# Attention inside a fused attention and MLP kernel: from split single-pass matmuls with transposes and repeated denominators to plain f32 matmuls on array tiles

## The chip, the cores and the metric

One core of a Trainium2 chip runs the whole program. The metric is the time of one execution on the device in microseconds (us), as the median of several executions. Less is better.

## What is computed

For 8 batches and 8 heads of 576 tokens with 64 values each, the reference computes an attention with 128 exponential features and their inverses, and then two MLP blocks:

```python
def phi(x):
    proj = np.einsum('bhsd,df->bhsf', x, w_phi)
    proj = proj - np.max(np.abs(proj), axis=-1, keepdims=True)
    return np.concatenate([np.exp(proj), np.exp(-proj)], axis=-1)
q_p, k_p = (phi(q), phi(k))
kv = np.einsum('bhsf,bhsd->bhfd', k_p, v)
z = np.sum(k_p, axis=2)
num = np.einsum('bhsf,bhfd->bhsd', q_p, kv)
den = np.einsum('bhsf,bhf->bhs', q_p, z)[..., None] + 1e-06
x = num / den                       # heads side by side: 8 x 576 x 512
# block 1: token shift with mu_k, mu_r; k = relu(xk @ w_k); v = (k * k) @ w_v; x = sigmoid(xr @ w_r) * v
# block 2: h = relu(x @ w_in); 3-tap convolution, sigmoid gate; out = (h * gate) @ w_out
```

All arrays are float32.

## The kernel before

**Two phases.** Phase 1 computes the attention and the first MLP block of all eight batches, and stores its result y to the chip's memory. Phase 2 (`phase_2`) reads it back and computes the second block. The change touches phase 1 alone.

**Numbers as pairs.** Nearly every large product is made of three matmuls (`three`): an operand is split into a high part of type f32r, which TensorE streams in one pass, and the low rest. Only the product of the keys' features with v (`sum_kv`, step KV) runs as plain f32.

**The attention of a pair of heads.** A batch has four pairs p. The steps of one pair are, by their letters in the lists of steps: T turns q and k (`turn`, ten TensorE transposes into the PSUM tensor `ps0`, then ACT writes the high and DVE the low part); QP and KP project q and k on all features with tokens on the partitions (`project`), and DVE takes the maxima of the magnitudes (`max_q`, `shift_k`; the second also subtracts them); M turns the split maxima of q into rows of `ps1` (`turn_maxima`), and ACT copies them; PA and PB make the features of q of one head each, with the features on the partitions, in `ps1` (`feature_rows`), and ACT takes both exponentials; SA and SB split them; EK takes the exponentials of k; KV sums the keys' features times v and 1; NA and NB multiply with the features of q (`attend`), again in `ps1`, where one row is the denominator. ACT copies numerator and denominator row out (`copy_num`).

**The denominators.** A row of 2 x 576 denominators goes by a transfer to a 128 x 9 tile, is inverted there (step RC, `invert`), goes to memory, and is read back repeated on 64 partitions for each head. Step DV (`divide`) multiplies on DVE and writes `x`.

**The first MLP block.** For each half of the tokens (288 of 576) there are 8 tiles K, 4 tiles R and 4 tiles V; a K or R tile is 12 matmuls, a V tile is two steps of 12 (`V-` and `V`). Their PSUM banks are the three of `psm`, in turn. Steps XK, HK, LK and XR, HR, LR mix and split x for them (group 0 is the first three pairs, group 1 the last pair).

**The order of the work.** Each engine runs one list of steps in order and waits on semaphores. `first_attention_steps` is the list for the first batch's attention, which has no MLP work beside it. `iteration` writes the list for one batch's MLP mixed with the next batch's attention: after an attention step it adds tiles worth so many ns (`FILL_NS`, `FIRST_FILL`, `TURN_FILL`) by the estimates of `PE_NS`; steps RC and DV follow NB by `RC_AFTER` and `DV_AFTER` ns of the same count, and are put in behind the step that passes that time. `batches` runs the first attention, one mixed iteration, a loop of six more, and the last MLP.

Of the kernel before, what the change touches and what calls it, by code (L numbers as in the profile page):

```python
# [11 lines left out]
P = 128  # L22
# [12 lines left out]
VW = D + 2  # L35
# [21 lines left out]
def attention_steps():  # L57

    steps = [("T", 0), ("QP", 0)]
    for p in range(PAIRS):  # L60
        more = p + 1 < PAIRS
        steps += [(s, p) for s in ("KP", "M", "EK", "PA", "SA", "KV", "PB")]
        steps += [("T", p + 1)] if more else []
        steps += [("SB", p), ("NA", p)]
        steps += [("QP", p + 1)] if more else []
        steps += [("NB", p)]
    return steps


def first_attention_steps():  # L70

    steps = [("T", 0), ("QP", 0), ("KP", 0)]
    for p in range(PAIRS):
        last = p == PAIRS - 1

        def ahead(s):
            return [(s, 0, "next") if last else (s, p + 1)]

        def before(s):
            return [(s, p - 1)] if p else []  # L80

        steps += [("M", p)] + before("RC") + [("PA", p), ("SA", p), ("EK", p)] + ahead("T")
        steps += [("PB", p)] + before("DV") + [("SB", p), ("KV", p)] + ahead("QP") + [("NA", p)]
        if not last:
            steps += ahead("KP") + [("NB", p)]
        else:
            steps += [("XK", 2, 0), ("NB", p), ("HK", 2, 0), ("LK", 2, 0), ("RC", p)]
            steps += [("XR", 2, 0), ("HR", 2, 0), ("LR", 2, 0)] + ahead("KP") + [("DV", p)]
    return steps + [(s + w, 2, 1) for w in "KR" for s in "XHL"]
# [6 lines left out]
def iteration(with_moe, with_next, ran_ahead=False):  # L96
# [38 lines left out]
    if with_next:  # L135
        fill(FIRST_FILL)
        for step in attention_steps():
            s, p = step[:2]
            if not (ran_ahead and step in (("T", 0), ("QP", 0), ("KP", 0))):
                emit(step)  # L140
            if with_moe:
                fill(FILL_NS.get(s, 0))
                if s == "NB":
                    later += [(now + RC_AFTER, ("RC", p)), (now + DV_AFTER, ("DV", p))]
                    later.sort(key=lambda t: t[0])
                if (s, p) in (("T", 0), ("PB", PAIRS - 1), ("NA", PAIRS - 1)):
                    fill(TURN_FILL * (2 if s == "NA" else 1))
        if with_moe:
            end = max(at for at, step in later if step[0] == "DV")
# [27 lines left out]
def build(nc, q, k, v, w_phi, mu_k, mu_r, w_k, w_v, w_r, w_in, conv_w, w_out, out):  # L177
    den_scr = nc.dram_tensor("den_scr", (PAIRS, 2, S), F32, kind="Internal").ap()
# [3 lines left out]
    with ExitStack() as ctx:  # L182
        early = phase_1(nc, ctx, q, k, v, w_phi, mu_k, mu_r, w_k, w_v, w_r, y_scr, den_scr, w_in)
# [26 lines left out]
def phase_1(nc, ctx, q, k, v, w_phi, mu_k, mu_r, w_k, w_v, w_r, y_scr, den_scr, w_in):  # L210
# [16 lines left out]
    phi_hi, phi_lo = sb_att("phi_hi", [P, 2, F], F32R), sb_att("phi_lo", [P, 2, F], F32R)  # L227
    ident = sb_att("ident", [P, P])
    pick = sb_att("pick", [P, 2, F], F32R)

    qk_nat = sb_att("qk_nat", [P, 2, TT, 2 * D])
    v_nat = sb_att("v_nat", [P, TT, 2, VW])
    qk_hi, qk_lo = sb_att("qk_hi", [P, 2, TT * P], F32R), sb_att("qk_lo", [P, 2, TT * P], F32R)
    q_max, k_max = sb_att("q_max", [P, TT, 2]), sb_att("k_max", [P, TT, 2])
    q_max_split = sb_att("q_max_split", [P, TT, 2, 2], F32R)
    max_rows = sb_att("max_rows", [P, TT * P], F32R)
    k_shift = sb_att("k_shift", [P, TT, 2, F])
    k_exp = sb_att("k_exp", [P, TT, 2, F])

    pick_f = k_exp[:, 0, :, :]  # L240
    phi = k_exp[:, 1, :, :]
    q_exp = sb_att("q_exp", [P, 2, S])
    q_exp_hi, q_exp_lo = sb_att("q_exp_hi", [P, 2, S], F32R), sb_att("q_exp_lo", [P, 2, S], F32R)
    kvz = sb_att("kvz", [P, 2, 2, 2 * D])
    kvz_hi, kvz_lo = sb_att("kvz_hi", [P, 2, 2, 2 * D], F32R), sb_att("kvz_lo", [P, 2, 2, 2 * D], F32R)
    num = sb_att("num", [P, S])
    den_row = sb_att("den_row", [1, 2, S])
    den_cols = sb_att("den_cols", [P, 2 * S // P])
# [32 lines left out]
    kv_summed, kvz_copied, kvz_hi_ready, kvz_lo_ready = sem("kv_summed"), sem("kvz_copied"), sem("kvz_hi_ready"), sem("kvz_lo_ready")  # L281
    features = sem("features")
# [946 lines left out]
```

## Time and profile before

| | us |
|---|---|
| median of the runs shown | 1486.46 (1486.41 to 1493.02) |
| span of the profiled execution, first to last instruction | 1483.8 |
| TensorE busy | 1416.3 (95%) |
| DVE busy | 818.5 (55%) |
| ACT busy | 797.9 (54%) |
| POOL busy | 14.4 (1%) |

The profiled execution has no time of its own beside its span; the median of the runs lies 2.7 us above that span. Matmuls are pipelined, so the busy time of one in a row counts its whole way through the array; how many fit in a microsecond is read from the distance between starts.

### The profile page before, as it was taken

How to read it: one execution, taken by the hardware profiler on the slowest of the kernel's cores; microseconds unless marked ns; L12 is line 12 of the kernel's file. 1: busy time of each engine (PE TensorE's matmuls, PEld its weight loads, DVE VectorE, ACT ScalarE, POOL GpSimd, SP SyncE). 2: the span in 40 equal slices, each digit the busy share in tenths (PEclk: the TensorE clock that was granted, in tenths of full speed). 3: DMA queues.
4: the chain of work that ended last, by engine and by line, in shares of the span. 5: the costliest groups of instructions: out<-in, count | busy, mean ns of one | idle time of the engine just before them, and what ended most of it. 6: DMA issues, size and time to landing. Idle time of an engine off the chain costs nothing. (4 is left out here: it accounts for less than half of the span.)

```text
span 1483.8 us, 26980 instructions
## 1 busy us (share of the span) xinstructions
PE 1416.3 (95%) x10240; PEld 1362.4 (92%) x10240; DVE 818.5 (55%) x1141; ACT 797.9 (54%) x1400; POOL 14.4 (1%) x20
## 2 busy tenths in 40 slices
PE   5778999999999999999999999999889999999998
PEld 5778999999999999999999999999879889988997
DVE  4565555554645564465555555554386468456653
ACT  4656674674666557466565746755244344344442
POOL 0000000000000000000000000000110000000000
PEclk9999999999999999999999999999999999999999
DMA  4412202211120221212122022121201110110101
GB/s 125 126 31 57 58 17 65 69 30 50 45 61 26 57 61 30 66 41 49 38 61 58 17 66 66 27 91 46 72 34 61 68 40 22 67 60 16 51 28 36
DMA packets 153461, 77.42 MB, mean 52 GB/s; under 512 B 131728, under 2 KB 140048, under 8 KB 152336
## 3 DMA queue, kind: packets, MB, share of 16 engines
q1 hardware_dynamic: 153360, 75.91, 18.5%
q8 instruction: 83, 1.36, 0.4%
q14 instruction: 18, 0.15, 0.0%
HBM read 56.71 MB, written 19.02 MB: 51 GB/s over the span
## 5 line engine op out<-in xcount | busy, mean ns | idle before, releaser
L512 PE MATMUL psm<-xk_hi,wk_hi 128*128 128x288 f32 x512 | 153.4, 300 | 16.5 <-DVE xk_lo L885 12.0
L1047 PE MATMUL psh<-y_hi,win_hi 128*128 128x288 f32 x512 | 154.0, 301 | 13.5 <-ACT h L1132 9.1
L1048 PE MATMUL psh<-y_lo,win_hi 128*128 128x288 f32 x512 | 152.5, 298 | 0.0
L512 PE MATMUL psm<-k_hi,wv_hi 128*128 128x288 f32 x512 | 152.1, 297 | 0.0
L1049 PE MATMUL psh<-y_hi,win_lo 128*128 128x288 f32 x512 | 151.9, 297 | 0.0
L512 PE MATMUL psm<-xk_lo,wk_hi 128*128 128x288 f32 x512 | 151.7, 296 | 0.0
L512 PE MATMUL psm<-xk_hi,wk_lo 128*128 128x288 f32 x512 | 151.2, 295 | 0.0
L512 PE MATMUL psm<-k_lo,wv_hi 128*128 128x288 f32 x512 | 151.1, 295 | 0.0
L512 PE MATMUL psm<-k_hi,wv_lo 128*128 128x288 f32 x512 | 150.8, 295 | 0.0
L890 DVE TENSOR_TENSOR k_lo<-square,k_hi 128x288 fp32r<-128x288 f32 x128 | 58.6, 458 | 156.1 <-ACT square L740 155.6
L1190 DVE SCALAR_TENSOR_TENSOR conv<-h,taps,conv 128x576 f32<-128x576 f32 x64 | 55.2, 863 | 141.7 <-ACT conv L1134 141.7
L844 DVE TENSOR_TENSOR q_exp_lo<-q_exp,q_exp_hi 128x1152 fp32r<-128x1152 f32 x60 | 81.5, 1359 | 88.4 <-ACT q_exp_hi L709 88.4
L512 PEld LDWEIGHTS psm<-xk_hi,wk_hi 128*128 128x128 f32 x512 | 96.8, 189 | 18.4 <-issue 10.1
L1047 PEld LDWEIGHTS psh<-y_hi,win_hi 128*128 128x128 f32 x512 | 97.2, 190 | 16.3 <-ACT h L1132 11.4
L1132 ACT ACTIVATE h<-psh 128x576 f32<-128x576 f32 x64 | 41.8, 653 | 129.6 <-DVE gated L1178 94.3
L1049 PE MATMUL pso<-wout_hi,g_lo 128*128 128x512 f32 x256 | 101.1, 395 | 0.0
L1047 PE MATMUL pso<-wout_hi,g_hi 128*128 128x512 f32 x256 | 101.0, 395 | 0.0
L1048 PE MATMUL pso<-wout_lo,g_hi 128*128 128x512 f32 x256 | 101.0, 394 | 0.0
L1048 PEld LDWEIGHTS psh<-y_lo,win_hi 128*128 128x128 f32 x512 | 97.5, 190 | 0.3
L1049 PEld LDWEIGHTS psh<-y_hi,win_lo 128*128 128x128 f32 x512 | 97.8, 191 | 0.0
L512 PEld LDWEIGHTS psm<-xk_hi,wk_lo 128*128 128x128 f32 x512 | 96.9, 189 | 0.0
L512 PEld LDWEIGHTS psm<-xk_lo,wk_hi 128*128 128x128 f32 x512 | 96.8, 189 | 0.0
(157 smaller groups left out, 3832.2 us busy)
## 6 DMA issues: line engine op xcount, KB each, us to landing
den<-den_scr SPq DMA_DIRECT2D x64, 144.0 KB, 3.0
y_scr<-y SPq DMA_DIRECT2D x64, 144.0 KB, 2.6
y<-y_scr SPq DMA_DIRECT2D x8, 1152.0 KB, 5.7
qk_nat<-in_q SPq DMA_DIRECT2D x64, 128.0 KB, 2.5
qk_nat<-in_k SPq DMA_DIRECT2D x64, 128.0 KB, 2.5
v_nat<-in_v SPq DMA_DIRECT2D x64, 128.0 KB, 2.5
out<-rows SPq DMA_DIRECT2D x32, 256.0 KB, 2.0
stage<-in_moe_w_in SPq DMA_DIRECT2D x4, 512.0 KB, 3.2
```

Of the source, the lines that this page charges most:

```text
L512: return nc.tensor.matmul(o, lhsT, rhs, start=first, stop=last)
L844: nc.vector.tensor_tensor(lo, q_exp[:], hi.bitcast(F32), ALU.subtract).then_inc(q_exp_lo_ready, 1)
L890: nc.vector.tensor_tensor(k2_lo[:, i, :], square[:, i % 2, :], k2_hi[:, i, :].bitcast(F32), ALU.subtract).then_inc(k2_lo_ready, 1)
L1047: nc.tensor.matmul(o, wh, xh, start=first, stop=False, skip_group_check=True)
L1048: nc.tensor.matmul(o, wh, xl, start=False, stop=False, skip_group_check=True)
L1049: return nc.tensor.matmul(o, wl, xh, start=False, stop=last, skip_group_check=True)
L1132: nc.scalar.activation(two(h[:, j % 2, 1:1 + S]), psh[:, j % 2, :, 0:HALF], ACT.Relu, scale=0.5).then_inc(h_ready, 1)
L1190: nc.vector.scalar_tensor_tensor(out=conv[:, j % 2, :], in0=h[:, j % 2, 0:S], scalar=taps[:, 0, j:j + 1], in1=conv[:, j % 2, :], op0=ALU.m ...
```

## The change

- q and k are handed to the program with the 2 x 64 values of a pair of heads on the partitions and tokens along them, and v in the layout of its tile (this is done to the arrays before the program starts). Step T goes, with the high and low parts of q and k. q and k have two buffers each (`qk`), and one transfer fills one.
- `project` uses plain f32 matmuls that contract over 64 partitions; the two heads lie on the two halves of the array's rows and alternate. `feature_rows` likewise, with P0 and P1 each for half of the tokens and both heads.
- The features of q and the sums kv and z are not split: SA, SB and the split of `kvz` go.
- A new step DEN (`sum_den`) multiplies z, read 64 times over as the stationary operand, with the features of q, so that the denominators come out repeated on 64 partitions, in `ps0`. NUM (`attend`) multiplies kv. In both, the two heads lie on the two halves of the array's columns and alternate.
- ACT copies the denominators to `den` (`copy_den`); DV is now a reciprocal of the whole 128 x 576 tile and the product, which reads the numerators from `ps1`. Both transfers of the denominators and step RC go.
- `ps1` becomes free for the next pair's M with DV (`x_ready`), where it was `num_copied` before.
- The list of steps, the fills and the estimates are new.

```diff
-PE_NS = {"T": 1100, "QP": 1600, "KP": 1600, "M": 500, "PA": 1000, "PB": 1000, "KV": 2200, "NA": 1500,
-         "NB": 1500, "K": 1480, "K-": 1110, "K+": 370, "R": 1480, "V-": 1480, "V": 1480}
-FILL_NS = {"QP": 1500, "M": 1500, "PA": 3000, "T": 2200}
-FIRST_FILL, TURN_FILL, RC_AFTER, DV_AFTER = 6000, 1500, 3500, 9000
+PE_NS = {"QP": 1100, "KP": 1100, "M": 550, "P0": 800, "P1": 800, "KV": 2240, "DEN": 1950, "NUM": 1950,
+         "K": 1590, "K-": 1190, "K+": 400, "R": 1590, "V-": 1590, "V": 1590}
+FILL_NS = {"QP": 2200, "M": 1600, "P0": 3500, "P1": 2600}
+FIRST_FILL, LAST_FILL, DV_AFTER = 11000, 1600, 700
...
 def attention_steps():
+    steps = [("QP", 0)]
     for p in range(PAIRS):
+        steps += [(s, p) for s in ("KP", "M", "EK", "P0", "KV", "P1", "DEN", "NUM")]
+        steps += [("QP", p + 1)] if p + 1 < PAIRS else []
     return steps
...
 def first_attention_steps():
+    steps = [("QP", 0), ("KP", 0)]
...
+        steps += [("M", p), ("P0", p), ("EK", p)] + ahead("QP")
+        steps += [("KV", p), ("P1", p)] + ahead("KP") + [("DEN", p), ("NUM", p), ("DV", p)]
+        if last:
+            steps[-1:-1] = [(s + w, 2, 0) for w in "KR" for s in "XHL"]
...
-                if s == "NB":
-                    later += [(now + RC_AFTER, ("RC", p)), (now + DV_AFTER, ("DV", p))]
+                if s == "NUM":
+                    end = now + DV_AFTER
+                    later += [(end, ("DV", p))]
...
+            for n in range(TT):
+                for h, t in ((0, (n - 1) % TT), (1, (n + 1) % TT)):
+                    own, b = slice(D * h, D * h + D), place(h, t)
...
+                    last = mm(ps[:, F * b:F * b + F], qk[own, p % 2, i, P * t:P * t + P], phi[own, :], True, True)
...
         def turn_maxima(p, a):
             await_(pe, q_max_split_ready, PAIRS, a, p + 1)
-            await_(pe, num_copied, 2 * H, a, 4 * p)
+            await_(pe, x_ready, PAIRS, a, p)
...
+            for h in range(2):
+                own = slice(D * h, D * h + D)
+                mm(ps1[:, BANK * h:BANK * h + HALF], phi[own, :], qk[own, p % 2, 0, cols], True, False)
+            for h in range(2):
+                own = slice(D * h, D * h + D)
+                last = mm(ps1[:, BANK * h:BANK * h + HALF], pick[own, :], max_rows[own, cols], False, True)
...
+        def sum_den(p, a):
+
+            await_(pe, kvz_copied, PAIRS, a, p + 1)
+            await_(pe, q_exp_ready, 2 * H, a, 4 * p + 4)
+            ps = att_psum(p, a)
             for n in range(2):
                 cols = slice(HALF * n, HALF * n + HALF)
                 for e in range(2):
+                    for h in range(2):
+                        last = mm(ps[D * h:D * h + D, BANK * (1 + n):BANK * (1 + n) + HALF],
+                                  kvz[:, h, e, D:D + 1].to_broadcast([P, D]), q_exp[:, e, h, cols], e == 0, e == 1)
+            last.then_inc(den_summed, 1)
+
+        def attend(p, a):
+
+            for n in range(2):
+                cols = slice(HALF * n, HALF * n + HALF)
+                for e in range(2):
+                    for h in range(2):
+                        last = mm(ps1[D * h:D * h + D, BANK * n:BANK * n + HALF], kvz[:, h, e, 0:D], q_exp[:, e, h, cols],
+                                  e == 0, e == 1)
             last.then_inc(attended, 1)
...
+        def copy_den(p, a):
+            await_(act, den_summed, PAIRS, a, p + 1)
+            await_(act, x_ready, PAIRS, a, p)
+            nc.scalar.activation(two(den[:]), halves(att_psum(p, a)[:, BANK:3 * BANK]), ACT.Copy, bias=1e-6).then_inc(den_copied, 1)
...
         def divide(p, a):
-            await_(dve, num_copied, 2 * H, a, 4 * (p + 1))
-            await_(dve, den_loaded, 32 * PAIRS, a, 32 * (p + 1))
-            nc.vector.tensor_tensor(x[:, p, 1:1 + S], num[:], den[:], ALU.mult).then_inc(x_ready, 1)
+            await_(dve, den_copied, PAIRS, a, p + 1)
+            nc.vector.reciprocal(den[:], den[:]).then_inc(inverted, 1)
+            await_(dve, inverted, PAIRS, a, p + 1)
+            await_(dve, attended, PAIRS, a, p + 1)
+            nc.vector.tensor_tensor(two(x[:, p, 1:1 + S]), halves(ps1[:]), two(den[:]), ALU.mult).then_inc(x_ready, 1)
```

## Rows read from the trace of the kernel before

**Rows 1.** The page: the span of the profiled execution.

```profile
span 1483.8 us, 26980 instructions
```

**Rows 2.** Stretches: length, busy PE, PEld, DVE, ACT, POOL, clock, DMA share, GB/s.

```profile
0.00:118.00 118.00, 79.23 (x567) 73.56 (x567) 67.85 (x77) 64.81 (x92) 3.49 (x16) 0.98 0.38 98
118.00:991.00 873.00, 862.15 (x6796) 855.05 (x6797) 470.88 (x666) 531.31 (x979) 0.00 (x0) 1.00 0.19 47
```

**Rows 3.** Timeline of DVE at the end of two iterations (start us, us).

```profile
350.16 0.45 DVE L897 SCALAR_TENSOR_TENSOR y<-gate,psm 128x288 f32<-128x288 f32 x1 [4.63 <-PE psm L512]
350.53 0.21 DVE L852 RECIPROCAL den_cols<-den_cols 128x9 f32<-128x9 f32 x1
350.66 1.00 DVE L885 TENSOR_TENSOR xk_lo<-mix,xk_hi 128x864 fp32r<-128x864 f32 x1
...
357.45 0.76 DVE L857 TENSOR_TENSOR x<-num,den 128x576 f32<-128x576 f32 x1 [0.48 <-DMA den<-den_scr]
...
482.87 0.75 DVE L857 TENSOR_TENSOR x<-num,den 128x576 f32<-128x576 f32 x1
```

**Rows 4.** Timeline of TensorE from an iteration's last V step into the next.

```profile
357.80 0.29 PE L512 MATMUL psm<-k_hi,wv_hi 128*128 128x288 f32 x1
...
359.25 0.29 PE L512 MATMUL psm<-k_hi,wv_lo 128*128 128x288 f32 x1
361.06 0.37 PE L512 MATMUL psm<-xk_hi,wk_hi 128*128 128x288 f32 x1 [1.51 <-DVE xk_lo L885]
```

**Rows 5.** Timeline of TensorE in an iteration: QP, M, KV and T begin and end.

```profile
401.99 0.28 PE L512 MATMUL ps<-phi_hi,qk_hi 128*128 128x256 f32 x1
...
403.78 0.71 PE L549 MATMUL ps<-ident,q_max_split 128*4 128x128 f32 x5
404.24 0.38 PE L512 MATMUL psm<-k_hi,wv_hi 128*128 128x288 f32 x1
404.46 0.29 PE L512 MATMUL psm<-k_lo,wv_hi 128*128 128x288 f32 x1
...
410.16 2.34 PE L512 MATMUL ps<-v_nat,k_exp 128*128 128x66 f32 x20
412.34 2.40 PE L512 MATMUL ps<-v_nat,k_shift 128*128 128x66 f32 x20
414.54 0.38 PE L512 MATMUL ps<-qk_hi,phi_hi 128*128 128x288 f32 x1
...
415.68 1.25 PE L527 MATMUL ps<-ident,qk_nat 128*128 128x128 f32 x10
416.69 0.38 PE L512 MATMUL psm<-k_hi,wv_hi 128*128 128x288 f32 x1
```

**Rows 6.** Groups of DVE by line and form: busy us, mean ns of one.

```profile
L822 DVE TENSOR_REDUCE q_max<-ps 128x10 f32<-128x1280 f32 x30 | 44.5, 1485 | 7.2 <-PE ps L512 7.2
...
L857 DVE TENSOR_TENSOR x<-num,den 128x576 f32<-128x576 f32 x32 | 24.1, 752 | 2.1 <-DMA den<-den_scr 2.1
...
L852 DVE RECIPROCAL den_cols<-den_cols 128x9 f32<-128x9 f32 x32 | 6.8, 211 | 15.0 <-DMA den_cols<-den_row 14.9
...
L826 DVE CAST q_max_split<-q_max 128x10 fp32r<-128x10 f32 x32 | 5.3, 164 | 1.6
```

**Rows 7.** Groups of ACT: the exponentials of q and of k.

```profile
L703 ACT ACTIVATE q_exp<-ps 128x576 f32<-128x576 f32 x128 | 75.2, 639 | 6.4 <-PE ps L512 6.4
...
L695 ACT ACTIVATE k_exp<-k_shift 128x1280 f32<-128x1280 f32 x32 | 40.6, 1268 | 28.9 <-DVE k_shift L837 28.9
```

**Rows 8.** Timeline of TensorE in the first attention: its start, two steps M, the first full tile.

```profile
8.68 2.37 PE L527 MATMUL ps<-ident,qk_nat 128*128 128x128 f32 x10 [8.68 <-DVE pick L806]
...
43.23 0.70 PE L549 MATMUL ps<-ident,q_max_split 128*4 128x128 f32 x5 [1.49 <-ACT num L730]
...
64.74 0.70 PE L549 MATMUL ps<-ident,q_max_split 128*4 128x128 f32 x5 [1.49 <-ACT num L730]
...
118.34 0.58 PE L512 MATMUL psm<-xk_hi,wk_hi 128*128 128x288 f32 x1 [5.47 <-DVE xk_lo L885]
```

More of the change, by code:

```diff
@@ L138, in iteration @@
             s, p = step[:2]
-            if not (ran_ahead and step in (("T", 0), ("QP", 0), ("KP", 0))):
+            if not (ran_ahead and step in (("QP", 0), ("KP", 0))):
                 emit(step)
@@ L142, in iteration @@
                 fill(FILL_NS.get(s, 0))
-                if s == "NB":
-                    later += [(now + RC_AFTER, ("RC", p)), (now + DV_AFTER, ("DV", p))]
+                if s == "NUM":
+                    end = now + DV_AFTER
+                    later += [(end, ("DV", p))]
                     later.sort(key=lambda t: t[0])
-                if (s, p) in (("T", 0), ("PB", PAIRS - 1), ("NA", PAIRS - 1)):
-                    fill(TURN_FILL * (2 if s == "NA" else 1))
+                if (s, p) == ("DEN", PAIRS - 1):
+                    fill(LAST_FILL)
         if with_moe:
-            end = max(at for at, step in later if step[0] == "DV")
             for at, which, g in ((end - X_AHEAD[0], "K", 0), (end - X_AHEAD[1], "R", 0), (end, "K", 1), (end, "R", 1)):
@@ L450, in work @@
                 of = attention_of(step, a)
[L451 removed]
+                if kind == "QP" and step[1] + 1 < PAIRS and step[-1] != "next":
                     load_qk(step[1] + 1, a)
[L453 removed]
+                elif kind == "QP" and step == ("QP", PAIRS - 1) and m is None:
                     load_qk(0, (None, 1))
@@ L456, in work @@
                     load_v(step[1] + 1, a)
-                if m is None and kind in ("QP", "KP", "PB") and pieces < len(PIECES):
+                if m is None and kind in ("QP", "KP", "P1") and pieces < len(PIECES):
                     load_piece(pieces)
@@ L498, in _ @@
                                 pattern=[[-1, P]], channel_multiplier=1).then_inc(ident_ready, 1)
-        for n, (part, h) in enumerate([(0, 0), (0, 1), (1, 0), (1, 1)]):
+        for n, row in enumerate((0, 1, D, D + 1)):
             pool.wait_ge(pick_made, 1 + n)
-            nc.gpsimd.affine_select(out=pick_f[:, h, :], in_=pick_f[:, h, :], compare_op=ALU.not_equal, fill=-1.0,
-                                    base=-(2 * part + h), pattern=[[0, F]], channel_multiplier=1).then_inc(pick_made, 1)
+            nc.gpsimd.affine_select(out=pick_f, in_=pick_f, compare_op=ALU.not_equal, fill=-1.0,
+                                    base=-row, pattern=[[0, F]], channel_multiplier=1).then_inc(pick_made, 1)
         pool.wait_ge(zeroed, 1)
@@ L723, in copy_num @@
-        def copy_num(h, p, a):
-            await_(act, attended, H, a, 2 * p + h + 1)
-            if h == 0:
-                await_(act, x_ready, PAIRS, a, p)
-                await_(act, den_spread, 16 * PAIRS, a, 16 * p)
-            own, row = (slice(D, P), slice(0, 1)) if h else (slice(0, D), slice(D, D + 1))
-            nc.scalar.activation(two(den_row[0:1, h, :]), halves(ps1[row, :]), ACT.Copy, bias=1e-6).then_inc(num_copied, 1)
-            nc.scalar.activation(two(num[own, :]), halves(ps1[own, :]), ACT.Copy).then_inc(num_copied, 1)
+            await_(act, attended, PAIRS, a, p)
```

322 lines of the change are left out of this document (96 added, 226 removed).

## The prediction

> **What bounds the kernel now.** I read the page first, then the stretches, then the timelines of DVE and TensorE, then the groups with their durations. The span is 1483.8 us [rows 1]; the median is 2.7 us above it, so I sum against the span and add 2.7 at the end. In the seven mixed iterations TensorE is busy 862 of 873 us at full clock, DVE 471 and ACT 531 [rows 2]: there only TensorE's own work or a wait put in its way moves the end. In the first attention it is busy 79 of 118 us: that stretch is a chain of short waits across the engines. Last V step to first K step of the next iteration leaves a hole of 361.06 - 359.25 = 1.8 us [rows 4]. Two DV steps of successive iterations lie 482.87 - 357.45 = 125.4 us apart [rows 3]; I call an iteration 126. Phase 2 is not touched: 0.
>
> **TensorE's work for a pair, before.** Twelve full f32r matmuls of 288 columns start from 357.80 to 359.25, eleven distances, so 0.132 each [rows 4]. QP: 403.78 - 401.99 = 1.8 for 15 matmuls; KP the same. M 0.46. KV 414.54 - 410.16 = 4.4. T 1.0 [rows 5]. PA and PB are 16 matmuls, 2.1; NA and NB 24, 3.2. Sum 3.6 + 0.5 + 4.4 + 1.0 + 2.1 + 3.2 = 14.8.
>
> **The same after.** The trace holds no plain f32 matmul on part of the array, and none longer than 66 columns. KV gives 4.38 / 20 = 0.22 us for one with 66 columns, in two recorded pieces (x20 for ten calls) [rows 5]. If KV is limited by its columns, 288 cost 0.22 x 288/66 = 0.96; if each piece is held up by loading its 128 columns of weights (0.11 each, and T also takes 0.10 for each 128-column load), the columns could be as cheap as four f32r passes, 4 x 0.132 = 0.53, a little less without the fixed part: 0.49. I take 0.49, since the transposes of M move 128 columns in 0.09 [rows 5], more than KV moves in a piece. For 128 columns, four passes give 0.22, and two weight loads 0.22 as well. Two tiles with disjoint rows or columns run side by side or one after the other: half of the sum or all of it. I take side by side, because their rows or columns share nothing; no row shows it, and the other end is a rival below. Then QP and KP: 10 x 0.22 / 2 = 1.1 each; P0 and P1: 0.49 plus one pair of f32r matmuls 0.13, 1.25 for both; DEN and NUM: 16 x 0.49 / 2 = 3.9; M 0.5, KV 4.4. Sum 12.2, which is 2.6 less.
>
> **Changing the shape of the tile.** Nine times in a pair TensorE changes between the whole array and half rows or half columns (into and out of QP, KP, P0, P1, DEN-NUM, less the neighbours). The nearest row is the change from f32 to f32r after M: 404.46 - 404.24 = 0.22 where 0.13 is normal, 0.09 more [rows 5]; the upper bound is an emptied array, a matmul's own 0.29 less the 0.13 distance, 0.16 [rows 4]. Nine times 0.09 to 0.16 is 0.8 to 1.4, less the three small changes there are now (0.3): 0.5 to 1.1; I take 0.7. If changes were free, 0.
>
> (The Trainium skill, TensorEngine Tiling (Array Packing), Key Properties, says that changing the tiling mode drains TensorE, and that tiles load weights and multiply in parallel. By the first the upper bound, 1.1, would hold, 11 us more over 28 pairs; by the second, side by side. No row here shows either.)
>
> So TensorE saves 2.6 - 0.7 = 1.9 us for a pair (from 1.5 to 2.6), and for 28 pairs in seven iterations **-53** (-42 to -73).
>
> **The reciprocal.** It is now of 576 elements in a partition. The trace has one of 9, 211 ns [rows 6]. A cast of 10 takes 164; products of 288 and 576 take 0.45 and 0.75 [rows 3, 6], 1.05 ns an element above about 155 fixed. So the nine elements account for 211 - 155 = 56 ns, 6.2 each, six times the product's. By starts instead: the reciprocal gives way after 350.66 - 350.53 = 0.13, and the product before it after 0.37 for 288, so 0.07 fixed and 7 each [rows 3]. For 576: 3.5 to 4.2; I take **3.6**. The bounds are far apart: if those 56 ns were only a longer fixed part, it would cost what the product costs, 0.75; if nothing were fixed, 211/9 x 576 = 13.5, excluded in effect, as every other small operation has the fixed part.
>
> **Where it stands.** By the new list DV(p) comes behind QP(p+1) (DV_AFTER 700 is below QP's 1100), so on DVE the maxima of q run first. Count from the end of NUM: QP 0.1 to 1.2; q_max 1.4 to 2.9 (1.49), its split to 3.3; reciprocal to 6.9; product to 7.7 [rows 6]. TensorE meanwhile does QP, one MLP tile of 1.6 (the fill of 2200 ns leaves one in pairs 1 to 3, as the debts of the earlier fills come out), KP, which waits for q_max at 2.9, until 4.2, and then stands at M, which now waits for `x_ready`: 3.6 us, as long as the reciprocal itself. Before, M waited for copies long done. Queued behind that M on TensorE are all MLP tiles, so the cover is gone. That is three times an iteration, 21 in all: **+76** (with 0.75: +16). Behind DV on DVE wait the low parts of the MLP tiles and k_max; k_shift ends about 11.1 and k's first exponential (1.27 on ACT [rows 7]) 12.5, still ahead of KV at about 14.
>
> **The end of an iteration.** Seven steps are left after the last NUM, 11.1 us. DVE does: y until 2.3; XK (one operation of 864 elements and three of 288, by the slope above 1.1 + 3 x 0.46), LK 1.0 [rows 3], XR, LR with ACT's high parts between, until 10.5; the reciprocal 14.1, product 14.9; XK of the last pair 15.9, and the y of V steps, behind all that, one of which frees the bank for the next iteration's first K step: 17.8. TensorE is there at 11.1: a wait of 6.7 in place of 1.8, seven times: **+34** (with 0.75: +14).
>
> **The first attention.** QP can start where T does, 8.7 [rows 8], or a little later, with two more DVE memsets; M follows at about 13.5, not 22.4, 9 saved. From M to M it takes 64.74 - 43.23 = 21.5 now. After: M and its copy 1.4, P0 0.8, exponentials of q 2 x 0.64 and of k 2 x 1.27 [rows 7] 4.0, second half of KV 2.3, P1 and KP 1.9, DEN 2.1, copy 0.7, reciprocal 3.7, product 0.9, and a weight split of 1.2 on DVE: 19. Three times 2.5 saved, and the end as late as before: **-15** (with 0.75 for the reciprocal -27).
>
> **What costs nothing.** ACT and DVE lose the splits of q, k, q_exp and kvz, and ACT the copies of the numerators; neither bounded the iterations (531 and 471 of 873 us [rows 2]), so this gives nothing by itself. The denominators' transfers were hidden behind the work that DV_AFTER, 9000 ns, puts before DV. The loads have two buffers and go one pair ahead.
>
> Sum: 1483.8 - 53 + 76 + 34 - 15 = 1525.8, with 2.7: **1528**.
>
> **Rivals.**
> *A cheap reciprocal: faster.* If the 9-element row is slow only in its fixed part, 0.75 replaces 3.6: -53 + 16 + 14 - 27 = -50, **1436**. For it: nothing in the trace separates latency from rate. Against it: two readings give 6 to 7 ns. It decides from about 1.9 us down, where the two stalls no longer eat the saving. Chance 0.28.
>
> *A still slower one.* Eight turns of the product's 1.05 ns for each element plus 0.15 make 5.0 us; the 28 waits grow by 1.4 each, the first attention by 6: 1528 + 45 = **1573**. The 9 elements would then take 76 ns and leave 135 fixed, a little less than any other row has. Chance 0.12. (The Trainium skill, VectorE: DVE Perf Modes, First, the fixed hardware budget, says that the reciprocal is an iterative division with a repeat count of 8; read as eight passes an element, this is its case, and the trace agrees to a factor of six or seven, not clearly of eight.)
>
> *The two tiles run one after the other, or f32 goes by KV's column rate.* Then 2.2 + 1.2 + 3.9 = 7.3 more for a pair, 205 for 28, of which 21 waits cover 1.1 each: 1528 + 182 = **1710**. For it: no row shows two matmuls at once. Chance 0.08.
>
> *Nothing to measure.* TensorE saves the full 2.6 and the reciprocal is 3.3 us or the waits overlap other ones: +76 and +34 lose 20, -53 becomes -73: **1487**. Chance 0.09.
>
> **Numbers.** The forecast has 0.43, and a range of its own of 1494 to 1565. A measurement of this kernel tells 0.5%, 7.4 us, from no change. Slower: 0.43 + 0.12 + 0.08 = 0.63; faster: 0.28; same: 0.09. The range from 1430 to 1575 takes in the cheap and the slower reciprocal, and leaves out the case of 1710 and the outer parts of the others.
>
> **What the profile after would show.** RECIPROCAL 128x576 near 3.6 us; idle time before M's matmuls, put down to DVE `x`, of 3 to 4 us, 21 times; DV to DV of successive iterations at about 132; starts of DEN's two heads nearly together, 8 pairs 0.49 apart; the first K step near 103. The forecast fails if the reciprocal is under 2 us, if DEN takes 3.9 instead of 1.95, or if TensorE is busy without holes.

## The result, and the profile after

| | before | after |
|---|---|---|
| median, us | 1486.62 (1486.41 to 1493.02, 4 runs) | 1646.99 (1642.95 to 1647.59, 4 runs) |
| span of the profiled execution, us | 1483.8 | 1645.1 |
| mean granted clock of TensorE | 0.995 | 0.923 |

The changed kernel is slower: ratio 1.1055, 95% interval 1.1027 to 1.1083, 160 us. The forecast had the sign and both new waits; it said 1528, with a range up to 1575, so 119 us are missing.

The page of the kernel after (span; busy time; the granted clock in 40 slices):

```profile
span 1645.1 us, 25897 instructions
...
PE 1463.7 (89%) x10368; PEld 1300.9 (79%) x10368; DVE 780.5 (47%) x1015; ACT 606.6 (37%) x1079; POOL 13.5 (1%) x18
...
PEclk8679899999989999999899999989999999999999
```

TensorE is busy 47 us longer than before, although the program has fewer matmuls (a plain f32 one is recorded as two pieces, so the x is no count of them). The clock row begins 8, 6, 7, 9, 8 and has an 8 in three more slices; a 9 is 90% or more and hides the rest, so shorter windows are needed (below). Groups by line and form (busy us, mean ns of one, idle time before them and what ended it):

```profile
L439 PE MATMUL psm<-xk_hi,wk_hi 128*128 128x288 f32 x512 | 173.7, 339 | 55.0 <-DVE y L778 47.5 <-DVE xk_lo L766 7.2 <-ACT relu L639 0.2
...
L439 PE MATMUL ps<-v_nat,k_exp 128*128 128x65 f32 x600 | 71.1, 274 | 5.9 <-ACT k_exp L615 5.9
...
L470 PE MATMUL ps<-ident,q_max_split 128*66 128x128 f32 x160 | 36.1, 383 | 91.5 <-DVE x L738 91.5
...
L735 DVE RECIPROCAL den<-den 128x576 f32<-128x576 f32 x32 | 119.9, 3746 | 0.0
```

The reciprocal takes 3.75 us (3.6 was forecast; [rows 6] had 211 ns for 9 columns, so (3746 - 211) / 567 = 6.2 ns an element between the two lengths, as worked out). M waits 91.5 us for it, of which 18.8 are in the first attention (5.96, 7.32 and 5.48), so 72.7 in the 21 places of the iterations: 3.5 each, where the forecast had +76 in all. The ends of the iterations wait 47.5 us for `y`, 6.8 each. Here is one of each, first on DVE and then on TensorE (start us, us; in brackets the idle time before and its releaser):

```profile
406.57 3.75 DVE L735 RECIPROCAL den<-den 128x576 f32<-128x576 f32 x1
410.35 0.76 DVE L738 TENSOR_TENSOR x<-ps,den 128x576 f32<-128x576 f32 x1
...
413.72 0.45 DVE L778 SCALAR_TENSOR_TENSOR y<-gate,psm 128x288 f32<-128x288 f32 x1
...
457.00 3.75 DVE L735 RECIPROCAL den<-den 128x576 f32<-128x576 f32 x1
460.78 0.76 DVE L738 TENSOR_TENSOR x<-ps,den 128x576 f32<-128x576 f32 x1
```

```profile
407.29 0.29 PE L439 MATMUL psm<-k_hi,wv_lo 128*128 128x288 f32 x1
414.41 0.58 PE L439 MATMUL psm<-xk_hi,wk_hi 128*128 128x288 f32 x1 [6.83 <-DVE y L778]
...
449.70 4.10 PE L439 MATMUL ps<-q_exp,kvz 128*64 128x288 f32 x32
453.74 1.39 PE L439 MATMUL ps<-phi,qk 64*128 64x128 f32 x20
455.05 0.40 PE L439 MATMUL psm<-k_hi,wv_hi 128*128 128x288 f32 x1
455.29 0.29 PE L439 MATMUL psm<-k_lo,wv_hi 128*128 128x288 f32 x1
...
456.83 1.39 PE L439 MATMUL ps<-phi,qk 64*128 64x128 f32 x20
461.68 1.25 PE L470 MATMUL ps<-ident,q_max_split 128*66 128x128 f32 x5 [3.46 <-DVE x L738]
462.58 0.59 PE L439 MATMUL psm<-k_hi,wv_hi 128*128 128x288 f32 x1
462.97 0.44 PE L439 MATMUL psm<-k_lo,wv_hi 128*128 128x288 f32 x1
463.21 0.44 PE L439 MATMUL psm<-k_hi,wv_lo 128*128 128x288 f32 x1
```

The reader should look past the two bracketed waits. M takes 0.90 us behind its wait (462.58 - 461.68) where it took 0.46 [rows 5], and the matmuls of the tile behind it start 0.24 apart (463.21 - 462.97) where full speed is 0.13 [rows 4]. The windows say why (length, busy PE, PEld, DVE, ACT, POOL, granted clock, DMA share, GB/s):

```profile
414.00:425.00 11.00, 10.59 (x64) 10.62 (x65) 2.37 (x6) 4.43 (x13) 0.00 (x0) 0.77 0.54 165
455.00:457.00 2.00, 2.00 (x18) 1.79 (x16) 1.76 (x4) 0.00 (x0) 0.00 (x0) 1.00 0.04 8
457.00:461.00 4.00, 1.22 (x20) 1.02 (x20) 3.97 (x3) 0.00 (x0) 0.00 (x0) 0.89 0.00 0
461.00:466.00 5.00, 4.32 (x19) 3.94 (x21) 3.58 (x4) 2.18 (x3) 0.00 (x0) 0.50 0.00 0
467.00:470.00 3.00, 3.00 (x25) 2.87 (x22) 0.00 (x0) 1.26 (x3) 0.00 (x0) 1.00 0.14 49
```

The clock is 1.00 ahead of the wait, falls near the end of it, is 0.50 (1.2 of 2.4 GHz) for the five us behind it, and 1.00 again from 467. The same is seen at the iteration's start (0.77 over 11 us), and behind each of the 28 waits in the iterations TensorE spends 3.2 to 5.8 us at half clock. So each wait is paid in two parts: once while TensorE stands, and again while it works at half speed behind it.

Since half a granted clock about doubles a step (0.90 for 0.46, 0.24 for 0.13), the loss is half of the time so spent. The iteration from 414.41 to the next such start at 561.20 is 146.8 us; in the kernel before it was 487.24 - 361.06 = 126.2. The spans differ by 161.3: 9.3 up to the first full K step (127.66 against 118.34 [rows 8]), 150.6 in the iterations and the last MLP, 1.4 in phase 2.

### The profile page after: what moved, and what is told of

Same layout as the page of the kernel before. It is cut to its first block and busy times, and to the rows that moved or that the text cites. A ratio compares the mean times of both kernels' runs of the same rounds, so it can differ in the third digit from the quotient of the medians.

```text
span 1645.1 us, 25897 instructions
## 1 busy us (share of the span) xinstructions
PE 1463.7 (89%) x10368; PEld 1300.9 (79%) x10368; DVE 780.5 (47%) x1015; ACT 606.6 (37%) x1079; POOL 13.5 (1%) x18
## 5 line engine op out<-in xcount | busy, mean ns | idle before, releaser
L439 PE MATMUL psm<-xk_hi,wk_hi 128*128 128x288 f32 x512 | 173.7, 339 | 55.0 <-DVE y L778 47.5
L920 PE MATMUL psh<-y_hi,win_hi 128*128 128x288 f32 x512 | 154.6, 302 | 13.5 <-ACT h L1005 9.1
L439 PEld LDWEIGHTS psm<-xk_hi,wk_hi 128*128 128x128 f32 x512 | 112.3, 219 | 64.1 <-issue 49.1
L778 DVE SCALAR_TENSOR_TENSOR y<-gate,psm 128x288 f32<-128x288 f32 x64 | 28.9, 451 | 261.3 <-PE psm L439 261.3
L439 PE MATMUL ps<-q_exp,kvz 128*64 128x288 f32 x992 | 129.6, 412 | 0.3 <-ACT q_exp L623 0.3
L735 DVE RECIPROCAL den<-den 128x576 f32<-128x576 f32 x32 | 119.9, 3746 | 0.0
L470 PE MATMUL ps<-ident,q_max_split 128*66 128x128 f32 x160 | 36.1, 383 | 91.5 <-DVE x L738 91.5
L639 ACT ACTIVATE relu<-psm 128x288 f32<-128x288 f32 x128 | 51.9, 405 | 167.6 <-PE psm L439 167.6
L439 PEld LDWEIGHTS psm<-xk_lo,wk_hi 128*128 128x128 f32 x512 | 112.0, 219 | 0.0
L439 PEld LDWEIGHTS psm<-k_hi,wv_hi 128*128 128x128 f32 x512 | 100.3, 196 | 14.0 <-issue 12.9
L439 PEld LDWEIGHTS ps<-q_exp,kvz 128*64 128x64 f32 x992 | 68.6, 137 | 48.2 <-issue 7.1
```

What stands on the lines that cost most here:

```text
L439: return nc.tensor.matmul(o, lhsT, rhs, start=first, stop=last)
L470: last = nc.tensor.transpose(ps1[0:ROWS, P * t:P * t + P], q_max_split[:, t, :, :].rearrange("p h r -> p (h r)")[:, 0:ROWS].bitcast(F32), ...
L639: nc.scalar.activation(relu[:, i % 2, :], psm[:, UNIT["K", n, i] % 3, 0:HALF], ACT.Relu).then_inc(k_relu, 1)
L735: nc.vector.reciprocal(den[:], den[:]).then_inc(inverted, 1)
L778: nc.vector.scalar_tensor_tensor(out=y[:, i % 2, :], in0=gate[:, i, :], scalar=1.0, in1=psm[:, UNIT["V", n, i] % 3, 0:HALF], op0=ALU.add, ...
L920: nc.tensor.matmul(o, wh, xh, start=first, stop=False, skip_group_check=True)
```

## The experiments

**1. Is it the clock?** This kernel keeps every wait of the kernel after, but gives TensorE work that nobody needs while it would stand at M: 26 f32r matmuls into the bank of the next MLP tile, in 21 places.

```diff
+        def stay_busy(rest, m, count):
+            kind, n, i = next(t for t in rest if t[0] in ("K", "R", "V-"))
+            t = (kind[0], n, i)
+            await_bank(pe, t, m)
+            for _ in range(count):
+                mm(psm[:, UNIT[t] % 3, 0:HALF], wk_hi[:, 0, 0:P], wk_hi[:, 1, 0:HALF], True, True)
...
                 elif kind == "M":
+                    if m is not None and step[1] > 0:
+                        stay_busy(steps[at + 1:], m, 26)
                     turn_maxima(step[1], of)
```

> The changed kernel with 26 needless f32r matmuls of 288 columns (3.4 us) on TensorE ahead of each M that waits for DV in the mixed iterations (21 places); they write a bank that the next tile overwrites. The waits for the reciprocal and for x stay as long as they are; only TensorE is no longer idle in them. Theory (the granted clock is the part that the prediction left out): M starts at the same moment, but the half-clock stretches behind these 21 waits vanish, which cost 2.4, 1.4 and 2.5 us an iteration: 44 us less than the changed kernel, near 1603. Rival (the time is in the waits alone, and the half clock costs nothing because other engines set the pace): 1647, or more by the matmuls.

Measured: 1593.69 (1588.43 to 1598.94), ratio 1.0714 (1.0618 to 1.0811). With 546 matmuls more, the kernel is 53 us faster than the one after. Its timeline of TensorE at one M:

```profile
471.77 3.69 PE L439 MATMUL psm<-wk_hi 128*128 128x288 f32 x26
475.30 0.71 PE L470 MATMUL ps<-ident,q_max_split 128*66 128x128 f32 x5
475.77 0.38 PE L439 MATMUL psm<-xk_hi,wk_hi 128*128 128x288 f32 x1
475.98 0.29 PE L439 MATMUL psm<-xk_lo,wk_hi 128*128 128x288 f32 x1
```

The 26 take 3.53 us, as long as the wait did; M is back at 0.47, and the tile behind it runs at full speed again, its matmuls 0.13 apart. From the first K step (116.95; 117.73 in the kernel after) to the first matmul of phase 2 the kernel takes 1054.9 us instead of 1101.5: the half clock behind 21 waits at M cost 46.6 us, 2.2 each. The rival's 1647 is out.

**2. The same in the kernel before.** If a wait is what costs, and not the change's matmuls, the old kernel must pay it too. DVE gets two needless maxima, 7.0 us together, behind q_max in pairs 1 to 3, and M waits for them.

```diff
                 elif kind == "M":
+                    if m is not None and step[1] > 0:
+                        await_(pe, delayed, 3, m, step[1])
                     turn_maxima(step[1], of)
...
                     max_q(step[1], of)
+                    if m is not None and step[1] > 0:
+                        await_(dve, delayed, 3, m, step[1] - 1)
+                        nc.vector.tensor_reduce(idle[:, 1:2], wk_hi[:].bitcast(F32), AX.XY, ALU.max)
+                        nc.vector.tensor_reduce(idle[:, 0:1], wk_lo[:, :, 0:575].bitcast(F32), AX.XY, ALU.max).then_inc(delayed, 1)
```

> The kernel before with 6.8 us of needless DVE maxima over weights behind q_max of pairs 1 to 3 in the mixed iterations, and M waiting for them; nothing else changed. By the old list some 5 us of TensorE's work lies between QP and M, so M waits about 3.7 us, 21 times. Theory (a wait costs itself and a stretch at half clock behind it): 1487 + 21 x (3.7 + 2.1) = 1610. Rival (a wait costs itself alone): 1487 + 78 = 1565.

Measured: 1632.58 (1630.37 to 1634.78), ratio 1.0976 (1.0916 to 1.1036). The waits came out longer than meant, 4.7 us each and not 3.7; the expectation's own sum is 1630 with them, and its rival's 1585. The group of M, and one window over the iterations, which is the second row of [rows 2] again:

```profile
L551 PE MATMUL ps<-ident,q_max_split 128*4 128x128 f32 x160 | 34.0, 367 | 102.9 <-DVE idle L920 98.4 <-ACT num L734 4.5
```

```profile
118.00:991.00 873.00, 779.06 (x5799) 765.58 (x5800) 522.73 (x605) 457.04 (x839) 0.00 (x0) 0.93 0.16 40
```

98.4 us of waiting made the work from the first K step to phase 2 1097.2 - 950.2 = 147.0 us longer: the clock of 1.00 fell to 0.93, and 104.5 us of TensorE's work ran at half speed where 2.8 did before. Half of the 101.7 is 51, and 98 + 51 = 149. In this kernel such a wait costs one and a half times itself, with none of the change in it.

**3. Take away the reciprocal's length.** It inverts 9 columns instead of 576. So that the product still has a sensible factor, the denominators are copied as 1: this kernel leaves out the division.

```diff
-            nc.scalar.activation(two(den[:]), halves(att_psum(p, a)[:, BANK:3 * BANK]), ACT.Copy, bias=1e-6).then_inc(den_copied, 1)
+            nc.scalar.activation(two(den[:]), halves(att_psum(p, a)[:, BANK:3 * BANK]), ACT.Copy, scale=0.0, bias=1.0).then_inc(den_copied, 1)
...
-            nc.vector.reciprocal(den[:], den[:]).then_inc(inverted, 1)
+            nc.vector.reciprocal(den[:, 0:9], den[:, 0:9]).then_inc(inverted, 1)
```

> The changed kernel with a reciprocal of 9 columns instead of 576, and denominators of 1 (scale 0, bias 1), so that the division is left out. Theory (reciprocal of 3.75 us, waits at M and at the iteration's end, and the clock behind them): the waits at M fall from 3.54 us to about 0.2, the end of an iteration from 7.1 to 3.5 us, and most half-clock stretches go: 21 x 3.4 + 7 x 3.6 = 97, clock 65, first attention 30: 1455, which is below the kernel before by the 32 us that TensorE saves. Rival (the new matmuls themselves make the kernel slow, through changes of the tile's shape): no faster than 1530.

Measured: 1472.56 (1471.32 to 1473.81), ratio 0.9900 (0.9852 to 0.9948). From the groups of this kernel:

```profile
L439 PE MATMUL psm<-xk_hi,wk_hi 128*128 128x288 f32 x512 | 161.2, 315 | 27.8 <-DVE y L778 23.3 <-DVE xk_lo L766 3.8 <-ACT relu L639 0.7
...
L470 PE MATMUL ps<-ident,q_max_split 128*66 128x128 f32 x160 | 25.1, 291 | 10.1 <-DVE x L738 10.1
...
L735 DVE RECIPROCAL den<-den 128x9 f32<-128x9 f32 x32 | 6.6, 207 | 0.0
```

The one operation, its waits and their clock are worth 174 us. But this is 17 us above what was expected of the run, and the kernel should then be the 1436 of the prediction's first rival, and is 37 slower. Half of that lies in the first attention: the first K step comes 8 us earlier than before (101.05 for 109.07), not 27, with 28.9 us of TensorE's work at half clock in place of 3.4. The other half lies behind it. The ends of the iterations still wait 3.3 us each (23.3 / 7), as an iteration's end is full of other DVE work. And TensorE's work saves less than forecast: from the first K step to phase 2 the kernel takes 946.4 us, 3.8 less than before, with 11.5 us more of waiting (3.6 of it KV's new wait for `k_exp`) and 9.6 more lost at half clock, so the work itself is some 25 us less, not 53.

**4. Give `ps1` free without waiting for the reciprocal.** ACT copies the numerators out (0.65 us), M waits for that copy, and DV multiplies from it.

```diff
-            await_(pe, x_ready, PAIRS, a, p)
+            await_(pe, num_copied, PAIRS, a, p)
...
+        def copy_num(p, a):
+            await_(act, attended, PAIRS, a, p + 1)
+            nc.scalar.activation(two(num[:]), halves(ps1[:]), ACT.Copy).then_inc(num_copied, 1)
...
-            await_(dve, attended, PAIRS, a, p + 1)
-            nc.vector.tensor_tensor(two(x[:, p, 1:1 + S]), halves(ps1[:]), two(den[:]), ALU.mult).then_inc(x_ready, 1)
+            await_(dve, num_copied, PAIRS, a, p + 1)
+            nc.vector.tensor_tensor(x[:, p, 1:1 + S], num[:], den[:], ALU.mult).then_inc(x_ready, 1)
```

> The changed kernel with ACT copying the numerators out of ps1 (0.65 us), and M waiting for that copy instead of DV, as it was before; the reciprocal stays as it is. Theory (what is wrong is where the reciprocal stands, in front of M): the 21 waits at M and their half-clock stretches go, 74 + 44; the end of the iteration stays with 7 us; in the first attention M no longer waits, 4 x 5: 1515 to 1535. Rival (DVE is the bottleneck, and the delay moves on to k_shift and KV): over 1600.

Measured: 1540.44 (1539.64 to 1541.24), ratio 1.0356 (1.0309 to 1.0404), 107 us better than after and 5 above the expected range. Its groups:

```profile
L441 PE MATMUL psm<-xk_hi,wk_hi 128*128 128x288 f32 x512 | 166.2, 325 | 55.8 <-DVE y L786 47.6 <-DVE xk_lo L774 8.1 <-ACT relu L645 0.2
...
L441 PE MATMUL ps<-v_nat,k_exp 128*128 128x65 f32 x600 | 72.4, 276 | 24.9 <-ACT k_exp L617 24.6
L472 PE MATMUL ps<-ident,q_max_split 128*66 128x128 f32 x160 | 25.1, 291 | 7.5 <-ACT num L640 7.5
```

The wait at M is gone (91.5 to 7.5). Part of it comes back one step later: M no longer stands, so KV arrives while the keys' exponential is late, held up on DVE by the same reciprocal (24.6 us instead of 5.9). The ends are as they were: a bank freed by `y` behind the reciprocal is not helped by a copy.

**5. Move the reciprocal in the list.** With that copy, DV has no one to hurry for. `DV_AFTER` 3500 puts it behind the next KP's DVE work; DV of the last pair goes straight behind NUM, and the first group's mixing, which stood ahead of it, behind KV and P1.

```diff
-FIRST_FILL, LAST_FILL, DV_AFTER = 11000, 1600, 700
+FIRST_FILL, LAST_FILL, DV_AFTER = 11000, 1600, 3500
...
-                    end = now + DV_AFTER
+                    end = now + (DV_AFTER if p + 1 < PAIRS else 0)
...
+                if (s, p) == ("KV", PAIRS - 1):
+                    mix("K", 2, 0, now)
+                if (s, p) == ("P1", PAIRS - 1):
+                    mix("R", 2, 0, now)
...
-            for at, which, g in ((end - X_AHEAD[0], "K", 0), (end - X_AHEAD[1], "R", 0), (end, "K", 1), (end, "R", 1)):
+            for at, which, g in ((end, "K", 1), (end, "R", 1)):
```

> e3_numcopy with another list: DV of pairs 0 to 2 behind the next KP instead of the next QP; DV of pair 3 straight behind NUM; and the mixes of group 0 for the next iteration behind KV and P1 of pair 3 instead of in front of DV. The same instructions. Theory (what is left is only where the reciprocal stands: ahead of k_shift, so ahead of KV, and ahead of the last y steps, and a stretch at half clock behind each wait): the waits of 1.6 and 1.9 us at KV and 5.3 of the 7.1 us at the iteration's end go; TensorE's own work is 4.2 us less an iteration than before, the first attention 18 less: 1440 to 1460, faster than the kernel before. Rival (DVE has too much to do in the iteration's end, wherever the reciprocal stands): over 1490.

Measured: 1448.85 (1443.96 to 1453.95), ratio 0.9739 (0.9697 to 0.9782): faster than both kernels. The reciprocal is as long as ever. Groups, and the turn of the loop on TensorE:

```profile
L445 PE MATMUL psm<-xk_hi,wk_hi 128*128 128x288 f32 x512 | 157.5, 308 | 15.7 <-DVE xk_lo L778 8.1 <-issue 5.3 <-DVE y L790 1.7
...
L476 PE MATMUL ps<-ident,q_max_split 128*66 128x128 f32 x160 | 24.6, 287 | 7.9 <-ACT num L644 7.9
...
L747 DVE RECIPROCAL den<-den 128x576 f32<-128x576 f32 x32 | 119.8, 3743 | 0.0
```

```profile
345.74 0.29 PE L445 MATMUL psm<-k_hi,wv_lo 128*128 128x288 f32 x1
347.35 0.37 PE L445 MATMUL psm<-xk_hi,wk_hi 128*128 128x288 f32 x1 [1.31 <-issue]
```

120 us of reciprocals now cost TensorE nearly nothing; the iterations run at a clock of 1.00 and take 122.4 us, with as much waiting in them as before (about 2 us). 126.2 - 122.4 = 3.8 an iteration is what the change's matmuls are worth. From the first K step to phase 2 it is 950.2 - 926.5 = 23.7, and 25 with the half clock taken out; that is less than 7 x 3.8, since the first iteration lacks QP and KP of its first pair. Experiment 3 gave 25 too.

**6. The reciprocal on GpSimd.** Experiment 4 with the inversion as a power of -1 on GpSimd, which has nothing else to do.

```diff
+                    nc.gpsimd.tensor_tensor(den[:], den[:], minus[:].to_broadcast([P, S]), ALU.pow).then_inc(inverted, 1)
...
-            nc.vector.reciprocal(den[:], den[:]).then_inc(inverted, 1)
```

> e3_numcopy with the reciprocal on GpSimd, as a power of -1, in place of DVE's; the product stays on DVE. Theory (the reciprocal on DVE is what makes KV and the iteration's end wait): if GpSimd takes up to some 5 us, the waits at KV vanish and the end of the iteration shrinks to 3.5 us: 1470 to 1490. If GpSimd is much slower, DVE waits for it in order and the kernel is slower than e3_numcopy's 1540; no row here tells its rate.

Measured: 4223.78 (4223.30 to 4224.25), ratio 2.84 (2.83 to 2.86). It is a dead end, and the groups say at what price:

```profile
L445 POOL TENSOR_TENSOR den<-den,minus 128x576 f32<-128x576 f32 x32 | 2951.0, 92220 | 766.1 <-ACT den L647 766.1
...
L739 DVE CAST q_max_split<-q_max 128x10 fp32r<-128x10 f32 x32 | 1853.3, 57916 | 1.6
```

One takes 92 us, 160 ns an element, against DVE's 6.2.

**7. Do the two tiles run side by side?** In the kernel after the heads alternate. Here DEN and NUM do one head and then the other.

```diff
-            for n in range(2):
-                cols = slice(HALF * n, HALF * n + HALF)
-                for e in range(2):
-                    for h in range(2):
+            for h in range(2):
+                for n in range(2):
+                    cols = slice(HALF * n, HALF * n + HALF)
+                    for e in range(2):
```

> The changed kernel with the loops of DEN and NUM turned: all matmuls of one head, then all of the other, so that neighbours use the same half of the array's columns. Theory (alternating heads run side by side): DEN and NUM take 7.8 us for a pair instead of 4.0, over 32 pairs some 120 us, so near 1765. Rival (the order does not matter, the halves overlap by whatever the array has in hand, or each matmul is cheap by itself): 1647.

Measured: 1683.37 in one run, so without an interval, 36 more than after. DEN and NUM take 5.16 us (461.78 to 466.94) instead of 4.03, which for 32 pairs is 36. That lies between the numbers expected, and the timelines of TensorE over a quarter of a microsecond show why. First this kernel early in DEN, where one head is at work, then the kernel after (x counts the pieces of the merged row that the window touches):

```profile
462.07 0.65 PE L439 MATMUL ps<-q_exp,kvz 128*64 128x288 f32 x2
```

```profile
450.00 0.66 PE L439 MATMUL ps<-q_exp,kvz 128*64 128x288 f32 x4
```

Two pieces in 0.65 us against four in 0.66. In this kernel the first pieces start at 462.075, 462.317, 462.560, 462.802: 0.243 for a piece of 288 columns on one tile. In the kernel after two start 6 ns apart and the next two 0.243 later, all through. So the tiles do run side by side, and a plain f32 matmul of 288 columns is two pieces, 0.486 us. That this kernel does not take the full 32 x 0.243 = 7.8 us shows in its trace too: from the sixth piece on, pieces start closer than one tile allows (distances of 0.006, 0.056 and 0.187). The records do not say which half of the array a piece is on, so it is inferred and not shown that TensorE takes up the second head before it is through with the first. By the time they take, turning the loops made it some 21 turns of 0.243 instead of 16, not 32.

**8. What does a change of the tile's shape cost?** Steps on full and on half rows or columns alternate nine times in a pair, and twelve times in the last pair of an iteration, where the list has a tile of the MLP between DEN and NUM and more of them behind NUM. On the version of experiment 5 one needless whole-array f32r matmul goes between DEN and NUM, and, as a control, the same one ahead of DEN, where TensorE is on the whole array anyway (the control has "DEN" for "NUM").

```diff
+        def whole_array(rest, m):
+            kind, n, i = next(t for t in rest if t[0] in ("K", "R", "V-"))
+            t = (kind[0], n, i)
+            await_bank(pe, t, m)
+            mm(psm[:, UNIT[t] % 3, 0:HALF], wk_hi[:, 0, 0:P], wk_hi[:, 1, 0:HALF], True, True)
...
+                if kind == "NUM" and m is not None:
+                    whole_array(steps[at + 1:], m)
```

> This is the version with the numerators copied out and the new list, with one needless f32r matmul of 288 columns on the whole array put between DEN and NUM in the 28 mixed pairs. Theory: in the kernel after, each change of the tile's shape costs about 0.2 us (0.1 on the way out of the last matmul of the old shape, 0.1 before the second of the new), not the 0.09 to 0.16 that the prediction took, and this is why TensorE saves 1.1 and not 1.9 us for a pair. Then DEN, the matmul and NUM take 4.03 + 0.13 + 2 x 0.2 = 4.56 us, an iteration 122.4 + 4 x 0.53 = 124.5, and the time is 1448.9 + 28 x 0.53 = 1464. Rival: a change costs 0.09, and the loss lies elsewhere: 4.03 + 0.13 + 0.18 = 4.34, an iteration 123.6, and 1457.

> The control of the run before: the same needless matmul, but ahead of DEN, behind a tile of the MLP, where TensorE works on the whole array anyway, so that no change of shape is added. Both theories expect 0.13 us for each of the 28, an iteration of 122.4 + 0.5 = 122.9 and 1452.6. If it costs as much as the matmul between DEN and NUM, the price there is not that of the shape but of the matmul or of the wait for its bank.

Measured: between them 1460.15 (1455.08 to 1476.20), ratio 0.9851 (0.9785 to 0.9918); ahead of DEN 1451.03 (1447.11 to 1462.88), ratio 0.9779 (0.9727 to 0.9830). The expectation counted two new changes in each of 28 pairs. In the last pair of each of the seven iterations the tile of the MLP already stands between DEN and NUM, so that there the matmul adds only itself: the theory then gives 1448.9 + 21 x 0.53 + 7 x 0.13 = 1461 and an iteration of 124.1, the rival 1456 and 123.5. The times scatter by more than that difference, so the traces decide. TensorE's timeline of the first:

```profile
498.63 2.16 PE L445 MATMUL ps<-q_exp,kvz 128*64 128x288 f32 x16
500.72 0.40 PE L445 MATMUL psm<-wk_hi 128*128 128x288 f32 x1
501.05 0.46 PE L445 MATMUL ps<-q_exp,kvz 128*64 128x288 f32 x2
```

By starts, DEN takes 2.09, the matmul 0.33, NUM 2.09, together 4.51 where DEN and NUM take 4.03, the same in all 21 pairs. The matmul itself is 0.13, which leaves 0.35 for two changes. In the control the stretch from the last matmul of the MLP to the next QP grows by 0.13 (4.38 for 4.25) and by nothing else. An iteration is 123.8 to 124.3 in three of four (the fourth has a stretch at half clock), and 123.2 in the control. With the waits taken out, an iteration is 121.9 us of work, 120.9 in the control and 120.4 without the matmul: 1.6 = 3 x 0.48 + 0.13 and 0.5 = 4 x 0.13.

## Why the prediction was wrong, by its own steps

**The step that failed: there was no term for the granted clock.** The prediction read "862 of 873 us at full clock" [rows 2] and went on with full-speed durations behind every wait that it had itself added. Of the 119 us that are missing, 62 are this term in the iterations, and so, by an estimate, are the 24 of the first attention; the saving of TensorE's own work, taken too large, is 28. Measured:

| term, iterations and last MLP | forecast | measured | from |
|---|---|---|---|
| TensorE's own work | -53 | -25 | experiments 3 and 5 |
| wait at M, 21 times | +76 | +73 | 91.5 - 18.8 |
| end of an iteration, 7 times | +34 | +37 | (7.0 - 1.7) x 7 |
| KV waits for `k_exp` | 0 | +4 | 3.6 of the 5.9 of its group; the rest is in the first attention |
| half clock behind M | 0 | +47 | experiment 1 |
| half clock behind an iteration's end | 0 | +15 | seven steps take 13.41 (414.41 to 427.82), 11.28 in experiment 5: 2.1 x 7 |
| sum | +57 | +151 | 150.6 by the trace |

The last line above the sum is a comparison of two traces, not tried by itself. The rows to find the term were in the trace of before, which has two stretches at half clock ahead of phase 2. One lies behind shorter waits (1.5 and 0.8 us, 64.74 and 66.23), the other behind the 5.47 us at 118.34 that [rows 8] shows, where the next matmul took 0.58, twice the 0.29 of [rows 4]. The windows of the kernel before around both, and two matmuls behind the second:

```profile
64.00:69.00 5.00, 3.47 (x18) 3.12 (x19) 1.79 (x2) 1.98 (x4) 0.00 (x0) 0.75 0.33 107
115.00:121.00 6.00, 2.66 (x11) 2.69 (x12) 3.90 (x8) 2.38 (x7) 0.00 (x0) 0.73 0.44 100
```

```profile
118.96 0.44 PE L512 MATMUL psm<-xk_hi,wk_lo 128*128 128x288 f32 x1
119.20 0.44 PE L512 MATMUL psm<-xk_hi,wk_hi 128*128 128x288 f32 x1
```

A forecast that adds 28 waits of 3.5 to 6.7 us to a loop that had none longer than 2.3 must ask what the clock did behind the longest one that the trace has. There the matmuls start 0.24 apart up to 121.12, which is 2.8 us, of which 1.4 are lost; 28 x 1.4 = 39 more would have given 1567, low still (2.2 and 2.1 were measured for each), but with the bound of the range moved in the right direction. (The Trainium skill, TensorE: Matmul & The Clock Gate, HAM oscillation — how this bites in real kernels, describes a loop whose every turn waits and so starts slow, and counts half of the slow time as lost. The trace agrees with both: the clock is back at 0.50 behind each wait, and experiment 2's 101.7 us of slow work account for 51 of its 147.)

**The reciprocal: right.** It took 3.75 where 3.6 was forecast, from nine columns' 211 ns at 6.2 ns an element. The rival of 0.75 and that of 5.0 are out.

**The two waits: right** in place, releaser and size, with their causes (experiments 3, 4 and 5 remove them one after the other). The other signs failed with the time: 132 us from DV to DV of successive iterations (its own terms give 134) became 146.8, and the first full K step, put near 103, came at 127.66.

**TensorE's steps: right one by one, wrong in what lies between.** Forecast and measured at full clock: QP or KP 1.1 and 1.31; P0 and P1 together 1.25 and 1.64; KV 4.4 and 4.5; DEN and NUM 3.9 and 4.03; M 0.5 and 0.49. 0.49 for a plain f32 matmul on a tile, two side by side, holds to the last digit (experiment 7), so the rival of 1710 is out. But 12.2 became 13.3, and the MLP tiles behind and ahead of these steps give another 0.7 for a pair (1.78 for a tile that was 12 x 0.13 = 1.58). Together 1.8 for nine changes of shape, 0.2 each, where 0.09 to 0.16 was taken; experiment 8 has 0.18. The term of 0.7 was 1.5 (1.8 less the 0.3 of before), and the saving 1.1 for a pair; the last pair has three changes more, which leaves the 3.8 an iteration of experiment 5. The row that stood for it, 0.09 from M to f32r [rows 5], was half of it: a change delays the first matmul of the new shape (449.48 to 449.70 into DEN, 0.22 for 0.13) and the second again (455.05 to 455.29, 0.24 for 0.13). The Trainium skill's rule that a change of mode drains TensorE (TensorEngine Tiling (Array Packing), Key Properties) goes the right way, as the measured 0.18 lies above the emptied array's 0.16; its other rule, tiles in parallel, is what experiment 7 shows.

**The first attention: wrong.** The forecast was -15, and +9 was measured. M of the first pair came early, at 12.17 (13.5 forecast). Then:

```profile
12.17 1.10 PE L470 MATMUL ps<-ident,q_max_split 128*66 128x128 f32 x5
39.24 1.25 PE L470 MATMUL ps<-ident,q_max_split 128*66 128x128 f32 x5 [5.96 <-DVE x L738]
...
68.98 1.25 PE L470 MATMUL ps<-ident,q_max_split 128*66 128x128 f32 x5 [7.32 <-DVE x L738]
91.55 1.25 PE L470 MATMUL ps<-ident,q_max_split 128*66 128x128 f32 x5 [5.48 <-DVE x L738]
```

From M to M it took 27, 30 and 23 us, with 19 forecast. Up to the first full K step 54.4 us of TensorE's work ran at half speed, 3.4 before; half of the difference is 25.5, the size of the 24 that are off. This is an estimate, as the stretch is a chain across the engines, and no experiment took the clock out of it. By the same halving the three distances would be 22, 21 and 20 at full clock, together 7 above the forecast, and the part behind the last M 25 where as much as before, 31, was taken: these two misses cancel, which is luck.

**Phase 2:** 0 forecast, 1.4 measured, below what can be told.

With the measured terms in place of the forecast ones: 1528 + 62 (clock in the iterations) + 28 (TensorE) + 24 (first attention) + 4 (KV's wait; those of M and of the ends cancel) + 1 = 1647, which is what was measured.

## What to carry to other kernels

A wait on the engine that sets the end costs more than itself when the clock falls behind it (3.5 us cost 5.7 here, 4.7 cost 7.0): look in the old trace for the longest idle stretch, read the granted clock and the distance of starts behind it, and price every new wait with that. An operation that has become long (here 0.2 to 3.75 us) need not be made shorter: it costs nearly nothing where it stands behind the small operations that others wait for and where its input buffer is freed by a copy. And many small steps in changing tile shapes pay at every change; count the changes like instructions.

## What the runs showed of the hardware

- Filling a wait with needless matmuls made the kernel faster: 546 f32r matmuls of 0.13 us, 72 us of work put into waits of 73, gave back 46.6 us of clock.
- DVE's reciprocal takes 207 ns for 9 columns and 3746 for 576, 6.2 ns for each more; no length between was run.
- GpSimd's power takes 160 ns an element. While it runs, some DVE operations stand: the cast of ten columns, 0.16 us in [rows 6], took 57.9 on average, though GpSimd works on another tensor. One that began at 940.66 ended at 1028.82, with the power that ran from 936.61 to 1028.79. What they share was not tried.
- A plain f32 matmul takes 0.22 us (two pieces at 0.11) with 128 columns on a tile of half the rows, and as much with 65 columns on the whole array; with 288 columns on a tile it takes 0.486. Two tiles' pieces start 6 ns apart.
- The clock in the first attention can differ between executions of the same list: three versions with the same first list (experiments 5 and 8) needed 100.2, 89.3 and 89.4 us up to the first K step, with 31, 10 and 8 us of work at half speed. So some 10 us between two profiles of such a stretch say nothing.
